# The state's product two groups later, and TensorE's loop over the middle batches written out, in a fused linear-attention and expert kernel

## What is computed

```python
# B, H, S, D = 4, 8, 768, 48; N = B * S = 3072 tokens of 384
for t in range(S):
    state = alpha[:, :, t, :, None] * state + einsum('bhd,bhe->bhde', k[:, :, t], v[:, :, t])
    y[:, :, t] = einsum('bhd,bhde->bhe', q[:, :, t], state)
x = y.transpose(0, 2, 1, 3).reshape(N, 384)
x = (sigmoid(x @ w_gate) * (x @ w_val)) @ w_out              # hidden size 1536
p = domain_probs / (domain_probs.sum(-1, keepdims=True) + 1e-9)
out = sum(p[:, e:e+1] * (maximum(x @ w1[e], 0) @ w2[e]) for e in range(4))   # hidden size 1024
```

## Time and profile before

| | |
|---|---|
| median of 3 runs | 1392.65 us |
| lowest and highest | 1389.51 and 1392.78 us |
| the profiled execution | 1386.33 us, its span 1384.5 us |
| TensorE busy in the span | 96% |
| VectorE, ScalarE, GpSimd busy | 62%, 54%, 70% |
| mean granted TensorE clock | 0.999 |

### The profile page before, as it was taken

The page is one execution under the profiler, slowest core; times in us unless marked ns, Lnnn a source line. Parts: engine busy times, 40 slices in busy tenths (PEclk is TensorE's granted clock), DMA queues, the critical chain, the costliest instruction groups (busy, mean ns, idle before and its releaser), DMA issues.

```text
span 1384.5 us, 33971 instructions
## 1 busy us (share of the span) xinstructions
PE 1334.9 (96%) x13162; PEld 1233.1 (89%) x13162; DVE 858.8 (62%) x1335; ACT 744.0 (54%) x1515; POOL 969.2 (70%) x942
## 2 busy tenths in 40 slices
PE   3889999999899999999999999999999999999998
PEld 2778999998899999998999999999989999999998
DVE  7685656656465656343666666666766666666666
ACT  6564645455455455346555555555755555555552
POOL 6686545545455547478889898987897777777772
PEclk9999999999999999999999999999999999999999
DMA  9413221312121312001010101010121010101001
GB/s 327 123 56 111 82 85 56 110 56 91 49 84 56 110 56 91 13 13 58 24 46 25 45 25 43 26 42 29 40 94 44 25 45 25 44 23 45 23 11 69
DMA packets 42429, 83.80 MB, mean 61 GB/s; under 512 B 5824, under 2 KB 31168, under 8 KB 42304
## 3 DMA queue, kind: packets, MB, share of 16 engines
q1 hardware_dynamic: 42304, 82.01, 18.6%
HBM read 77.28 MB, written 4.72 MB: 59 GB/s over the span
## 4 chain that ended last, share of the span: by engine, by line
PE 78%; issue 7%; POOL 6%; DMA 4%; DVE 3%; ACT 1%; SPq 1%; POOLq 0%; DVEq 0%; ACTq 0%
PE PS L872 28%; PE PS L861 24%; PE PS L756 14%; PE PS L766 7%; DMA V<-in_v 3%; POOL row L1487 1%; PE PS L697 1%; POOL TOT L1470 1%; PE PS L726 1%; PE PS L722 1%; DVE KQ L1186 1%; POOL row L1480 1%; POOL hs1l L1510 1%; POOL hs0l L1510 1%; POOL y_near L1493 1%
## 5 line engine op out<-in xcount | busy, mean ns | idle before, releaser
L1426 DVE SCALAR_TENSOR_TENSOR acc<-PS,prob,acc 128x384 f32<-128x384 f32 x360 | 221.9, 616 | 209.5 <-PE PS L872 209.5
L967 ACT ACTIVATE QX<-KQ 48x256 f32<-48x256 f32 x288 | 120.7, 419 | 127.6 <-DVE KQ L1186 104.1
L1088 ACT ACTIVATE mixed<-PS 128x512 f32<-128x512 f32 x192 | 112.6, 589 | 89.8 <-PE PS L861 89.0
L1186 DVE TENSOR_TENSOR KQ<-KQ,TOT 112x512 f32<-112x512 f32 (+1 forms) x126 | 116.8, 951 | 36.0 <-PE PS L706 11.9
L1279 DVE TENSOR_TENSOR hid<-PS,hid 128x384 f32<-128x384 f32 x96 | 53.4, 556 | 126.1 <-PE PS L756 112.9
L1116 ACT ACTIVATE mixed<-mixed 128x512 f32<-128x512 f32 x192 | 118.4, 617 | 0.0
L1510 POOL TENSOR_TENSOR hs1l<-hid,hs1h 128x384 fp32r<-128x384 f32 x48 | 55.4, 1154 | 77.8 <-ACT hs1h L986 77.8
L1510 POOL TENSOR_TENSOR hs0l<-hid,hs0h 128x384 fp32r<-128x384 f32 x48 | 55.1, 1148 | 67.2 <-ACT hs0h L986 67.2
L1115 ACT ACTIVATE H_1h<-mixed 128x512 fp32r<-128x512 f32 x32 | 20.3, 634 | 130.5 <-DVE mixed L1400 130.5
L697 PE MATMUL PS<-QX,KQ 112*32 112x32 f32 x3072 | 48.8, 204 | 34.7 <-ACT QX L967 20.3
L697 PEld LDWEIGHTS PS<-QX,KQ 112*32 112x32 f32 x3072 | 41.0, 116 | 43.3 <-issue 27.1
(11 more groups left out here) (538 smaller groups left out, 4971.3 us busy)
## 6 DMA issues: line engine op xcount, KB each, us to landing
row<-in_rows SPq DMA_DIRECT2D x24, 768.0 KB, 4.4
KQ<-in_qka SPq DMA_DIRECT2D x24, 672.0 KB, 4.7
rawA<-in_w SPq DMA_DIRECT2D x32, 384.0 KB, 3.1
rawB<-in_w SPq DMA_DIRECT2D x32, 384.0 KB, 3.2
V<-in_v SPq DMA_DIRECT2D x24, 384.0 KB, 4.9
out_y<-acc SPq DMA_DIRECT2D x24, 192.0 KB, 2.6
raw<-in_w_gate SPq DMA_DIRECT2D x3, 768.0 KB, 13.9
raw<-in_w_val SPq DMA_DIRECT2D x3, 768.0 KB, 13.5
```

Source lines behind the costliest of these rows:

```text
L967: done = nc.scalar.activation(QX[p][rows, :, g, :].rearrange("d a (n t) -> d a n t", t=2 << level), right, ACT.Copy)
L1088: nc.scalar.activation(mixed[:, COPIED[g], :], PS[:, hidden_banks[HIDDEN[g]], :], ACT.Copy).then_inc(copied, 1)
L1186: dve.tensor_tensor(x, x, y, ALU.mult).then_inc(kq_ready[p], 1)
L1426: dve.scalar_tensor_tensor(out=to, in0=result, scalar=weight, in1=to, op0=ALU.mult, op1=ALU.add).then_inc(acc_ready, 1)
```

## The change

In both lists of slots STATE moves from the slot of YOUT to the end of the slot of TRX, two dense groups later, behind level 3 of the next step and ahead of PREP. DVE's scaling of the old state becomes a task of its own, SCALE, that stays in YOUT's slot, behind level 2 of the next step; the other engines skip it. The banks follow the new order by themselves. In SP's queue the wait for the state's product leaves `load_step` and stands in `load_rows`, between the loads of row and of V. TensorE's loop over batches 1 and 2 is written out; the loops of the other engines stay.

```diff
@@ attention_slots
             if level == LEVELS:
-                tasks += [(YOUT, j, 0), (STATE, j, 0)]
+                tasks.append((YOUT, j, 0))
...
             if level == LEVELS:
                 slots[at(n) + 2].insert(0, (TRX, j, 0))
+        for j in range(STEPS_T):
+            level = n - 4 * j + AHEAD
+            if level == LEVELS:
+                tasks.append((SCALE, j, 0))
+            if level == LEVELS + 1:
+                tasks.append((STATE, j, 0))
         slots[at(n)] += tasks
+    slots[at(4 * STEPS_T - 1) + 2].append((STATE, STEPS_T - 1, 0))
     return slots
@@ before_in_bank
-        if in_use(kind, sc % CHUNKS):
+        if in_use(kind, sc % CHUNKS) and not (isinstance(i, int) and CHUNKS * i + sc >= STEPS):
@@ SP load_step
                     wait_count(sp, y_done, per_step(i, sc - 2, 1, 1))
-                    wait_count(sp, state_done, per_state(i, sc - 2, 1 if (sc - 2) % CHUNKS < CHUNKS - 1 else 0))
@@ SP load_rows
+                    if to is V[buffer_of(i, sc)] and not is_first(i, sc):
+                        wait_count(sp, state_done, per_state(i, sc - 2, 1 if (sc - 2) % CHUNKS < CHUNKS - 1 else 0))
@@ TensorE
-            with pe.Fori(1, B - 1) as i:
+            for i in range(1, B - 1):
                 tile(i, 0)
                 tile(i, 1)
@@ VectorE
+            def scale_state(i, sc):
+
+                dve.wait_ge(*decays_done(i, sc, LEVELS))
+                dve.tensor_tensor(ST[0:R], ST[0:R], tot_of(i, sc, C)[0:R].to_broadcast([R, PAIRS, 2 * D]),
+                                  ALU.mult).then_inc(state_scaled, 1)
...
+                if kind == SCALE:
+                    if exists(i, sc) and in_use(STATE, sc) and chunk:
+                        scale_state(i, sc)
+                    return
...
                     if chunk:
-                        dve.wait_ge(*decays_done(i, sc, LEVELS))
-                        dve.tensor_tensor(ST[0:R], ST[0:R], tot_of(i, sc, C)[0:R].to_broadcast([R, PAIRS, 2 * D]),
-                                          ALU.mult).then_inc(state_scaled, 1)
+                        if not base:
+                            scale_state(i, sc)
                         dve.wait_ge(state_scaled, per_scaled(i, sc))
```

More of the change, by code:

```diff
@@ L76 @@
 LVL, TRK, YOUT, STATE, TRX = "level", "transpose k", "y", "state", "transpose y"
-PREP = "prepare"
+PREP, SCALE = "prepare", "scale"
 AHEAD = 3
@@ L114 @@
 FIRST_SLOTS = attention_slots(True)
-SEQUENCE = [task for slot in SLOTS for task in slot if task[0] != PREP]
+SEQUENCE = [task for slot in SLOTS for task in slot if task[0] not in (PREP, SCALE)]
 ATT_BANKS = 3
@@ L129 @@
 assert len(FIRST) % ATT_BANKS == len(LEAD) % ATT_BANKS == len(SEQUENCE) % ATT_BANKS == 0
-assert [task for slot in FIRST_SLOTS for task in slot if task[0] != PREP][AHEAD:] == SEQUENCE
+assert [task for slot in FIRST_SLOTS for task in slot if task[0] not in (PREP, SCALE)][AHEAD:] == SEQUENCE
 def is_first(i, sc):
@@ L681, in task @@
                 p, chunk = buffer_of(i, sc), sc % CHUNKS
-                if kind == PREP or not in_use(kind, sc) or not exists(i, sc):
+                if kind in (PREP, SCALE) or not in_use(kind, sc) or not exists(i, sc):
                     return
@@ L922, in task @@
                     return
-                if kind == PREP:
+                if kind in (PREP, SCALE):
                     return
```

## The result

The changed kernel takes 1378.95 us, the median of 6 runs (1373.43 to 1382.09), and the kernel before, measured beside it, 1390.59 us. The ratio is 0.9913, with a 95% interval of 0.9892 to 0.9934: faster by 9 to 15 us. The profiled execution takes 1375.55 us instead of 1386.33, 10.8 us less.

The account below looks back on a forecast made before the run. TensorE, busy 96% of the span, was taken to bound the kernel, so only its idle or slow stretches could pay. 5.2 + 5.85 + 0.4 - 0.3 - 1.3 = 9.85 us off 1392.65 gave 1382.8 us, range 1378.7 to 1389.2.

Parts of the forecast that it names:

- The loop's turn, 5.2 us: Where TensorE's loop turns, ahead of tile (2,0): writing it out removes two gaps and a slow clock, saving 5.2 us once.
- rival 2: The turn's cost stays because DVE, ACT or POOL turn late: 5.2 us less saved, 1388.0 us; chance 0.05.
- Six gaps, 5.85 us: TensorE's stops for late code inside bursts of 160 pairs: shortened to 128 by moving STATE, all go, saving 5.85 us.
- 0.3 us for gaps in bursts of 128: Allowance for a code packet ending badly in TensorE's bursts of 128 pairs: costs 0.3 us, bounds 0 and 2.8.
- Rival 1: Gaps come back elsewhere as code moves against the packets' ends: half of 5.85 us returns, 1385.7 us; chance 0.12.
- Rival 3: The six gaps inside bursts aren't code and stay, by the skill page's rule: saving 4.3 us, 1388.3 us; chance 0.05.
- VectorE's adds, 1.3 us: Adds between level 3 and PREP delay level 0's queries in slot 23 and the first tile: costs 1.3 us, bounds 0 to 2.7.
- The queries of level 3, 0.4 us: With level 3's queries earlier on DVE, TensorE's waits right behind TRX in two places go, saving 0.4 us.
- SyncE, 0: SP's wait for the product, moved from KQ's load to ahead of V, costs 0, at most 0.2 us.
- Rival 4: DVE is held by the product at the adds, making each PREP late: 4.3 us slower, 1396.9 us; chance 0.04.

Follow-up runs that it names:

- shift of 192: The changed kernel with 192 more TensorE instructions, a repeated task of small matmuls, at the start of tile (0,1): 1387.19 us in a single run.
- shift of 96: The kernel before with TensorE's loop written out and 96 more TensorE instructions at the start of tile (0,1): 1388.43 us in a single run.
- the last run: The changed kernel with SyncE's wait for the state's product back in front of the load of KQ: 1425.06 us in a single run.

## Why the prediction was right or wrong

The forecast was 1382.8 us with a saving of 9.85 on the profiled execution; measured were 1378.95 us and 10.8. The direction was right, and the size of the profiled saving to a tenth (by the medians, 11.6 us, it was under by 1.8); the time lies at the low end of the range, partly as the kernel before itself measured 1390.59 us in the wider set of runs, not 1392.65.

**The loop's turn, 5.2 us: right.** Kept in an otherwise changed kernel it costs 5.6 us in tile (2,0), 3.2 of them gaps. Written out, that tile is 0.66 us longer than (1,0), where the forecast allowed 0.5; it holds the gap of 0.74. That the other engines' turns stay hidden held too (rival 2).

**Six gaps, 5.85 us: the amount nearly right (0.7 us is left), late code the right cause, the rule that a burst of 128 pairs is safe wrong.** The failed step is "all 32 matmuls of its level 2 follow each other without a gap, in each of its three places". It was read from one place. The first gap in the earlier trace rows stands in another of the three, slot 8 of tile (0,1), the batch's first chunk, a burst of 64 + 32 + 32 = 128 pairs: the trace of before held the counterexample, listed as a case of the rule that it breaks. Its products of YOUT and STATE, with 21 of level 2's 32 behind them before the stop:

```profile
153.06 0.89 PE L726 MATMUL PS<-V,AT 128*32 128x48 f32 x64
153.77 0.53 PE L735 MATMUL PS<-V,Kn 128*32 128x48 f32 x32
```

What the runs showed in its place: a burst stops where its code comes late, at 128 pairs too (0.76 us here, 0.74 in the changed kernel, 1.42 and 1.78 in other runs), and a shorter burst is only hit less. Nor do the 5.85 us belong to the move alone. The loop alone, with all its long bursts, removed four of the six gaps (5.9 us of gaps before, 3.7 with it); the move alone, with the loop kept, removed all but 0.2 us. Behind the loop the move is worth 3.0 us of gaps, ahead of it 5.7.

**0.3 us for gaps in bursts of 128: mis-sized.** 0.5 to 0.7 us in the two profiles of the change, 1.7 with a shift of 192, inside the bounds of 0 to 2.8.

**Rival 1 (gaps elsewhere) had the mechanism.** Gaps do depend on where packets end, and the one that was left stood in a new place. It failed in the amount, half of 5.85: 0.7 us came.

**Rival 3, and the Trainium skill's rule.** The gaps are code: they moved when TensorE's code was shifted by a task repeated, and each ends 2.2 to 3.0 us after a code packet's start. The page "Runtime: NRT & Kernel Launch" of the Trainium skill, section "Instruction fetch mechanics", has crossing a block of code mostly hidden. For dense groups of 0.17 us a matmul these traces agree but for the first few matmuls behind a burst (1.48 us ahead of the first and 0.43 us ahead of the ninth with the shift of 96); for bursts of 15 ns a matmul they don't, by up to 1.6 us a time in the six tiles. The section of the Trainium skill also says that a taken branch to code that isn't loaded waits until this has come. The turn agrees: its two stops of 0.87 and 2.58 us end 2.6 and 2.3 us after a packet's start.

**VectorE's adds, 1.3 us: mis-sized.** In slot 23 TensorE waited once for 0.2 us, in the first tile its waits were the 4.0 us of before. Two things were left out. Level 4 ahead of level 0 still runs when level 0 could start, in the place above for 0.14 us more. And in the first tile VectorE's instructions around the adds took other times than before, together less. Its timeline in slot 16 there, before and then after:

```profile
93.15 0.92 DVE L1186 TENSOR_TENSOR KQ<-KQ,TOT 112x512 f32<-112x512 f32 x1
94.00 1.51 DVE L1195 TENSOR_TENSOR TOT<-KQ 112x256 f32<-112x256 f32 x1
```

```profile
93.29 1.29 DVE L1194 TENSOR_TENSOR KQ<-KQ,TOT 112x512 f32<-112x512 f32 x1
94.50 0.71 DVE L1281 TENSOR_TENSOR ST<-ST,PS 48x192 f32<-48x192 f32 x2
95.24 0.77 DVE L1203 TENSOR_TENSOR TOT<-KQ 112x256 f32<-112x256 f32 x1
```

From the start of level 3 to the end of PREP's first instruction it was 2.36 us and is 2.72: with the adds in between only 0.36 us more, which the moved product's 0.34 us covers. Why the same instructions took other times was not tried.

**The queries of level 3, 0.4 us: right,** no wait behind TRX is left. **SyncE, 0: right** for the change as it stands, but incomplete, as the last run shows. **Rival 4** stayed as far away as the trace had it.

Outside the six tiles the first 138 us took 0.5 us more and the experts, whose code is the same, 0.8 less. I can't tell these from the differences between executions.

## What to carry to other kernels

When an engine stops inside a task with no wait in it, look at the queue that loads code before looking at semaphores, then shift the code by some instructions in front of it: a gap that moves speaks for late code. In this kernel bursts of very short instructions and the turn of a long loop are where it happened, so writing out a long loop that runs few times and putting long instructions between bursts are worth a try. Before giving a gain to an edit, list every place that has the supposed harmless shape, not one; and before moving work later, follow what waits for it on the transfer queue to the first user of the data that is loaded behind it.

## What the runs showed of the hardware

**Code reaches TensorE in packets of 16 KB, and a burst can outrun them.** From the start of a packet in the trace to the first product behind the gap went 2.2 to 3.0 us (323.54 to 325.96). The gaps lasted from 0.2 to 1.6 us in the six tiles, and up to 3.5 us in the first steps of attention. The loop of two tiles loads its code again in each pass (20 packets in either, 19 in the same tiles written out) and has 3.2 to 3.5 us of gaps at its turn. The experts' loops on TensorE turn without a gap; between 810 and 989 us of the kernel before, that queue has no packet at all.

**The clock follows idling, but not every idling.** After 1.37 us it stayed at 2.4 GHz; after the turn it was 1.2 GHz for 3.4 us in the kernel before and 6.8 us in the changed one with its loop kept, and the mean of the tile 0.98 and 0.96. In the last experiment's run TensorE waited eleven times for 2.1 to 3.1 us: after four of the waits, of 2.1 to 2.4 us, the clock was at half for 3.4 us, and after the longest, 3.07 us, it stayed at 1.00. So the length of a single stop doesn't tell. From 365.30 us, behind that longest wait, and from 445.80 us, behind one of 2.27 us:

```profile
365.30:368.70 3.40, 3.40 (x50) 3.27 (x41) 3.00 (x4) 2.62 (x9) 2.02 (x3) 1.00 0.03 10
445.80:449.10 3.30, 3.30 (x12) 3.30 (x11) 2.65 (x4) 2.88 (x9) 2.38 (x3) 0.50 0.00 0
```

Much of the difference between profiled executions lies at the start of the kernel, where TensorE waits often. The execution of the kernel with the loop kept, 0 to 144.11 us, and the changed one, 0 to 138 us:

```profile
0.00:144.11 144.11, 109.22 (x2177) 98.48 (x2181) 97.56 (x162) 80.72 (x186) 90.24 (x99) 0.95 0.46 148
```

```profile
0.00:138.00 138.00, 102.94 (x2158) 92.43 (x2158) 97.53 (x161) 80.83 (x186) 91.30 (x99) 1.00 0.48 155
```

The same work up to the end of the first tile took 144.1 us at a mean clock of 0.95, with a gap of 1.78 us in it, and 138.3 us at 1.00. That is over half of what the change gains, and the reason why the comparison here goes by tiles.

**Parts of a change that remove the same gap don't add:** 8.2 and 5.5 us alone, 10.4 together.
